# Chunked attention ahead of two MoE layers: step-by-step order on TensorE, masks made on TensorE, k and v on a second queue

## The reference

```python
def _attn_ref(q, k, v):                     # 4 batches, 8 heads, 768 tokens, 64 dims
    gamma = 1.0 - 2.0 ** (-5.0 - np.arange(H)); scale = 1.0 / np.sqrt(D)
    for t in range(S):
        state = gamma * state + outer(k[:, :, t], v[:, :, t])
        y[:, :, t] = scale * (q[:, :, t] @ state)
def _moe_ref(x, w_a, w_b, w_out):           # 3072 x 512, d_ff 1536
    return ((x @ w_a) * (x @ w_b)) @ w_out
def _moe2_ref(x, ...):                      # 8 experts, top-1 routing, d_ff 1024
    out[mask] = gate * eom * (relu(x[mask] @ w1[e]) @ w2[e])
```

## Time and profile before

| | us |
|---|---|
| median of 3 runs | 1030.78 (1030.44 to 1032.24) |
| the profiled execution | 1030.35 |
| its span, first to last instruction | 1028.5 |
| PE busy in it | 1012.5 (98%) |
| DVE, ACT, POOL busy | 553.4, 283.7, 120.2 |

### The profile page before, as it was taken

The page is one execution under the profiler, slowest core; times in us unless marked ns, Lnnn a source line. Parts: engine busy times, 40 slices in busy tenths (PEclk is TensorE's granted clock), DMA queues, the critical chain, the costliest instruction groups (busy, mean ns, idle before and its releaser), DMA issues.

```text
span 1028.5 us, 17407 instructions
## 1 busy us (share of the span) xinstructions
PE 1012.5 (98%) x5761; PEld 841.5 (82%) x5762; DVE 553.4 (54%) x1211; ACT 283.7 (28%) x490; POOL 120.2 (12%) x108
## 2 busy tenths in 40 slices
PE   6999999999999999999999999999999999999998
PEld 5898888888888888888888878888888888888886
DVE  3455342487567747773877323466554635354642
ACT  2554331221212122112211212131533424333431
POOL 4870000000000000000000000001211111211211
PEclk9999999999999999999999999999999999999999
DMA  9998700511061114103310312021754334254311
GB/s 365 368 322 264 198 1 1 144 58 46 1 158 47 41 32 133 52 31 82 93 52 21 83 41 81 2 62 41 288 178 142 134 109 164 88 175 156 114 42 37
DMA packets 53865, 114.37 MB, mean 111 GB/s; under 512 B 8749, under 2 KB 23405, under 8 KB 53296
## 3 DMA queue, kind: packets, MB, share of 16 engines
q1 hardware_dynamic: 48752, 98.95, 30.4%
q0 software_dynamic: 4480, 13.91, 4.0%
q10 hardware_dynamic: 576, 0.79, 0.2%
HBM read 96.81 MB, written 17.61 MB: 111 GB/s over the span
## 4 chain that ended last, share of the span: by engine, by line
PE 98%; DMA 1%; issue 0%; SPq 0%; DVE 0%; POOL 0%; ACT 0%; DVEq 0%; POOLq 0%
PE bank L1078 38%; PE bank L1109 19%; PE bank L1442 15%; PE bank L1466 14%; PE bank L1450 2%; PE bank L606 2%; PE bank L559 2%; PE bank L671 1%; DMA rows<-in_steps 1%; PE bank L593 1%; PE bank L573 1%; PE bank L1165 0%; PE bank L985 0%; PE bank L852 0%; PE bank L1151 0%
## 5 line engine op out<-in xcount | busy, mean ns | idle before, releaser
L1078 PE MATMUL bank<-x_hi,wab_hi 128*128 128x512 f32 x576 | 224.5, 390 | 0.0
L1078 PE MATMUL bank<-x_hi,wab_lo 128*128 128x512 f32 x576 | 224.1, 389 | 0.0
L1078 PE MATMUL bank<-x_lo,wab_hi 128*128 128x512 f32 x576 | 224.1, 389 | 0.0
L1007 DVE SCALAR_TENSOR_TENSOR products<-y_sb,gate_row 128x512 f32<-128x512 f32 x256 | 176.9, 691 | 23.7 <-DMA gate_row<-xT_dram 16.4
L1442 PE MATMUL bank<-w,xe 128*128 (+1 forms) x648 | 158.9, 399 | 0.5 <-DVE xe L695 0.5
L1442 PEld LDWEIGHTS bank<-w,xe 128*128 128x128 f32 x648 | 119.4, 188 | 28.1 <-issue 1.8
L1019 DVE TENSOR_TENSOR g_sb<-bank,b_sb 128x512 f32<-128x512 f32 x72 | 49.7, 690 | 168.2 <-PE bank L1078 168.2
L1078 PEld LDWEIGHTS bank<-x_hi,wab_hi 128*128 128x128 f32 x576 | 108.2, 188 | 22.8 <-issue 0.3
L1078 PEld LDWEIGHTS bank<-x_lo,wab_hi 128*128 128x128 f32 x576 | 108.2, 188 | 22.4
L1078 PEld LDWEIGHTS bank<-x_hi,wab_lo 128*128 128x128 f32 x576 | 108.1, 188 | 22.4
L1109 PE MATMUL bank<-wo_hi,g_hi 128*128 128x512 f32 x288 | 113.4, 394 | 0.0
(11 more groups left out here) (172 smaller groups left out, 1067.7 us busy)
## 6 DMA issues: line engine op xcount, KB each, us to landing
raw<-in_w SPq DMA_DIRECT2D x64, 512.0 KB, 6.1
gate_row<-xT_dram SPq DMA_DIRECT2D x64, 256.0 KB, 3.2
rows<-in_steps SPq DMA_DIRECT2D x20, 768.0 KB, 7.9
rows<-in_steps SPq DMA_DIRECT2D x24, 256.0 KB, 7.2
wab_raw<-in_weights SPq DMA_DIRECT2D x24, 256.0 KB, 8.5
x_rows<-y_sb SPq DMA_DIRECT2D x6, 1024.0 KB, 9.0
xT_dram<-x_all SPq DMA_DIRECT2D x4, 1024.0 KB, 11.9
x_raw<-xT_dram SPq DMA_DIRECT2D x16, 256.0 KB, 8.2
```

Source lines behind the costliest of these rows:

```text
L1007: nc.vector.scalar_tensor_tensor(products, y_sb[:, t], 1.0, gate_row[e % GATE_SLOTS], ALU.mult, ALU.mult, accum_out=L3[:, t, e:e + 1]).the ...
L1078: ins = nc.tensor.matmul(to, wab(w, f, j), x[s][:, k, :], start=(k == 0 and m == 0), stop=(k == KD - 1 and m == 2))
```

## The change

- TensorE's order in a round of steps f and s is now: scores f, kv f, scores s, within f, kv s, within s, then cross of the round. There is no look-ahead and no `first_up`; all 24 first products of the dense layer follow the last round.
- VectorE's order is now per step: probabilities, then the new state. ScalarE decays the state per step, then evicts. GpSimd's order is per step: decay k, decay q; q's buffer is taken again once the round three before is done with everything, not only with `cross`.
- kv alternates between two banks (6 and 7); the waits for slots and for v are per step.
- The masks are no longer loaded (512 KB). Two products of 4 rows by 128 and 4 rows by 512 columns make all powers of the decays in banks 4 and 5, and VectorE multiplies them with a triangle (64 KB, loaded) into `mask_t`. Before them, TensorE runs two 512-column products on zeros.
- First load: SP brings only qT and kT of the first six steps (512 KB each), ScalarE's queue k and v (512 KB each), behind the powers, the triangle and `kdec_t`; `qdec_t` goes in behind k, v of step 1. ScalarE then runs one small activation on `kdec_t`.

```diff
@@ pe_attention @@
-        scores(0, 0, True)
-        kv(0, 0, True)
         with pe.Fori(0, B) as b:
             for j in range(RB):
-                if j < RB - 1:
-                    scores(b, j + 1)
-                    kv(b, j + 1)
-                else:
-                    with pe.If(b < B - 1):
-                        scores(b, RB)
-                        kv(b, RB)
-                    with pe.If(b > B - 2):
-                        first_up()
-                cross(b, j)
-                within(b, j)
+                first, second = ROUND * j, ROUND * j + 1
+                scores(b, first)
+                kv(b, first)
+                scores(b, second)
+                within(b, first)
+                if second < CH - 1:
+                    kv(b, second)
+                within(b, second)
+                cross(b, j)
...
+        pe.wait_ge(zeros_done, 1)
+        for _ in range(2):
+            nc.tensor.matmul(bank[7], probs[0][:, 0, 0, :], probs[0][:, 0, 0:PAIRS].rearrange("p a t -> p (a t)"), start=True, stop=True)
+        for o in range(2):
+            four = slice(o * D, o * D + PAIRS)
+            pe.wait_ge(pow_in[o], 16)
+            nc.tensor.matmul(bank[4 + o], pow_t[four, 0:P], pow_t[four, P:], start=True, stop=True).then_inc(mask_made[o], 1)
@@ dve_attention @@
+        def masks():
+            dve.wait_ge(triu_in, 16)
+            for o in range(2):
+                dve.wait_ge(mask_made[o], 1)
+                nc.vector.tensor_tensor(mask_t[o], bank[4 + o].rearrange("p (a t) -> p a t", a=PAIRS),
+                                        triu.unsqueeze(1).to_broadcast([P, PAIRS, P]), ALU.mult).then_inc(mask_done, 1)
...
-                probabilities(b, j)
-                new_states(b, j)
+                for c in range(ROUND * j, ROUND * j + ROUND):
+                    probabilities(b, c)
+                    if c < CH - 1:
+                        new_state(b, c)
@@ act_attention @@
+            act.dma_start(pow_t[four], const_in[four, C_POW:C_POW + POW]).then_inc(pow_in[o], 16)
+        act.dma_start(triu, const_in[:, C_TRIU:C_QDEC]).then_inc(triu_in, 16)
+        act.dma_start(kdec_t, const_in[:, C_KDEC:C_TRIU]).then_inc(kdec_in, 16)
+        for c in range(CH):
+            kinds = slice(2 if c < CH - 1 else 3, 4)
+            act.dma_start(rows[:, c, kinds], steps_in[c][:, kinds]).then_inc(v_in[c], 16)
+            if c == 1:
+                act.dma_start(qdec_t, const_in[:, C_QDEC:C_POW]).then_inc(qdec_in, 16)
...
-                if r + 1 < ROUNDS:
-                    decayed_states((r + 1) // RB, (r + 1) % RB)
+                if ROUND * j + 1 < CH - 1:
+                    decayed_state(b, ROUND * j + 1)
+                if j < RB - 1:
+                    decayed_state(b, ROUND * j + 2)
                 evict(b, j)
@@ sp_attention @@
+        for c in range(CH):
+            sp.dma_start(rows[:, c, 0:2], steps_in[c][:, 0:2]).then_inc(qk_in[c], 16)
+        for n in range(STEPS - CH):
+            if n > 0:
+                sp.wait_ge(v_read, n)
+                load_v(n - 1 + CH)
+            if n % CH < CH - 1:
+                sp.wait_ge(kv_done, kvs_until(n))
+            else:
+                sp.wait_ge(scores_done, n + 1)
+            if n % CH > 0:
+                sp.wait_ge(q_dec_done, n // CH * (CH - 1) + n % CH)
+            load_qk(n + CH)
@@ pool_attention @@
+                if c < CH - 1:
+                    k = rows[:, c, 2].rearrange("p (h d) -> p h d", h=H)
+                    pool.wait_ge(v_in[c] if b == 0 else qk_in[c], (b + 1) * 16)
...
-                    pool.wait_ge(cross_done, r - RB + 1)
+                        pool.wait_ge(attn_done, round_no(b - 1, j) + 1 + CREDIT)
```

More of the change, by code:

```diff
@@ L407, in sp_attention @@
         load_wab(sp, 0)
-        sp.wait_ge(attn_done, ROUNDS - RB + CREDIT)
-        for i in range(ROUND):
-            load_v(ROUNDS - 1, i)
+        sp.wait_ge(v_read, STEPS - CH)
+        load_v(STEPS - 1)
         load_wo(sp, 0)
@@ new lines, in pe_attention, with scores @@
+        pe.sem_inc(state_new, CREDIT)
+        pe.sem_inc(probs_done, ROUND)
+        def scores(b, c):
+            i = c % ROUND
+            pe.wait_ge(qk_in[c], 16 * b + 16)
+            pe.wait_ge(probs_done, CH * b + c + 1)
+            qT, kT = rows[:, c, 0], rows[:, c, 1]
+            for p in range(PAIRS):
+                for o in range(2):
+                    half_p, cols = slice(o * D, (o + 1) * D), slice(p * P, (p + 1) * P)
+                    ins = nc.tensor.matmul(bank[2 * i + o][:, cols], kT[half_p, cols], qT[half_p, cols], start=True, stop=True)
+            ins.then_inc(scores_done, 1)
@@ new lines, in kv @@
+        def kv(b, c):
+            pe.wait_ge(state_new, (CH - 1) * b + max(c - 1, 0) + CREDIT)
+            pe.wait_ge(k_dec_done, (CH - 1) * b + c + 1)
+            pe.wait_ge(v_in[c], 16 * b + 16)
+            pe.sem_inc(cross_ready, 1)
+            for h in range(H):
+                p, o, cols = h // 2, h % 2, slice(h * D, (h + 1) * D)
+                ins = nc.tensor.matmul(bank[6 + c % ROUND][o * D:(o + 1) * D, p * D:(p + 1) * D],
+                                       rows[:, c, 2, cols], rows[:, c, 3, cols], start=True, stop=True)
@@ L596, in cross @@
-            ins.then_inc(cross_done, 1)
-        def within(b, j):
-            for i, c in chunks(j):
-                pe.wait_ge(probs_done, CH * b + c + 1)
-                if c == CH - 1:
-                    pe.wait_ge(v_in[c], 16 * b + 16)
-                for a in range(0, PAIRS, 2):
-                    for p, o in ((a, 0), (a + 1, 0), (a, 1), (a + 1, 1)):
-                        h = 2 * p + o
-                        ins = nc.tensor.matmul(out_at(i, p, o), rows[:, c, 3, h * D:(h + 1) * D], probs[j][:, i, h, :],
-                                               start=False, stop=(i == ROUND - 1 and p >= PAIRS - 2), skip_group_check=True)
-            ins.then_inc(attn_done, 1)
@@ L1114, in group @@
             for f in range(KF):
-                pe_up(pe, g, s, f, (0,) if first and f == 0 else (1, 0))
+                pe_up(pe, g, s, f)
                 if first and f == 0:
```

210 lines of the change are left out of this document (81 added, 129 removed).

## The result

The changed kernel takes 1037.37 us (median of 5 runs, 1036.01 to 1038.42). The kernel before, in five runs beside it, took 1030.78 us (1030.44 to 1032.24). The ratio is 1.006, with a 95% interval of 1.0045 to 1.0074: slower, by 6.6 us. The profiled execution took 1037.5 us, its span is 1035.7. Against the profile of before that is 7.2 us more.

The account below looks back on a forecast made before the run. The prediction took TensorE's order to bound the kernel, with the start waiting for DMA. Start -1.1 and steady rounds +5.2 gave +4.1 us on the profiled 1030.35, 1034.5 there and 1034.9 as median; range 1031.2 to 1039.5.

Parts of the forecast that it names:

- the steady rounds: Attention rounds 3 to 11: a batch takes 18.82 us against 17.09, three times, +5.2 us.
- The start: Up to the end of round 2: it ends at 30.3 us against 31.4, a gain of 1.1 us.
- seam: From attention to the dense layer: no gain, no loss; ScalarE may block 2 us on the first dense weights.
- the 0.21 us from the end of a VectorE instruction to TensorE: In each round: delay from the end of VectorE's probs until TensorE can use them, 0.21 us.
- forecast stall: Before a round's second within: TensorE waits 0.26 us for probs, 0.72 us in a batch's last round.
- the landing of k 0: At the start: k of step 0 lands near 9.6 us behind 384 packets, so kv 0 starts at 10.85.
- turns of one for one: In the first loads: while both DMA queues have work, they take turns packet by packet, 89 against 89.
- rival 1: At the start: second queue brings k and v in time, start gains 5.1 us, 1031.0 us, no change; chance 0.19.
- The masks by products: At the start: zeros and mask products end at 6.6 to 8.3 us, none of it on the path.
- rival 2: Steady rounds: on top of an early start, only the fifth group change is paid, 1.4 us; 1027.1 us; chance 0.07.
- rival 3: Rounds 0 and 1: TensorE may stay at 1.2 GHz, costing 2.5 to 4.5 us; 1037.4 to 1039.4 us; chance 0.13.
- Records at 62 ns from scores 0 on: At the start: sign named beforehand that TensorE's products run at 62 ns a piece from scores 0 on.

Follow-up runs that it names:

- a_extra_dve: The changed kernel with one more VectorE instruction of 128 x 512 behind the first step's work of each round 0 to 8: 1040.48 us.
- a_all_on_sp: The changed kernel with all first loads of q, k and v on SP, as in the kernel before, ScalarE's queue having only the constants: 1033.93 us.
- a_masks_loaded: The changed kernel with the two masks loaded at the head of ScalarE's queue, without powers, triangle and the products on zeros and powers: 1035.71 us.
- b_masks: The kernel before with only the masks made by products (zeros, powers, triangle); q, k and v stay on SP's queue: 1031.21 us.
- best: The changed kernel with each kind's two steps side by side, first loads on SP, `kdec_t` first, dense weights asked for sooner, low half split later: 1027.11 us.

## Why the prediction was right, and where it was off

The forecast was 1034.9 us, slower, from 1031.2 to 1039.5. The measured 1037.37 lies inside, 2.5 us above the forecast. The sum was +4.1 us on the profile, the profile shows 7.2. The direction is right by its largest term, the steady rounds. The start came out with the wrong sign, and only the width of the range holds it. By its terms:

| term | forecast | measured |
|---|---|---|
| start, to the end of round 2 | -1.1 | +1.4 |
| rounds 3 to 11 | +5.2 | +4.3 |
| seam | 0 | +0.8 |
| behind the transpose | 0 | +0.7, scatter |

**Steady rounds: mechanism right, size 0.9 too large.** Rounds of 5.88, 6.32 and 6.32 us stand against 5.98, 6.42 and 6.42. VectorE's chain sets them, as a_extra_dve shows, and scores f to probs s is as long as worked out. The term that was mis-sized is the 0.21 us from the end of a VectorE instruction to TensorE. It was read off one place at the start; here it is 49.27 - 49.21 = 0.06 us. Also, kv s between the two `within` takes 0.54 us and not 0.46, so part of the forecast stall is work.

**Start: the failed step is the landing of k 0.** The prediction counted 384 packets of ScalarE's queue up to k 0 and took the time that 384 had taken in the kernel before, 9.6 us. With the two loads of powers, 16 packets, the count is 400, which changes little. What was wrong is the pace. By 5 us ScalarE's queue had sent 16 packets, against 102 before, while SP's had sent 193 against 114; by 9 us ScalarE's had 320 against 442. The turns of one for one began only after 5 us. So `kdec_t` was there at 9.7 us, no sooner than before, with 272 packets up to it in place of 384, and k 0, 128 packets of 4 KB behind it, landed at 12.3.

The empty stretch is not a price of the half rows: a_all_on_sp, with whole rows on SP, has the same 16 packets by 5 us. With masks in place of the small loads (a_masks_loaded) ScalarE's queue had sent 143 by 5 us, and k 0, with 112 packets more ahead of it, came as late: GpSimd began at 12.44 us, against 12.40. Why the small loads leave their queue so empty stays open. With the loads on SP kv 0 comes at 10.72 us, forecast 10.85, and round 2 ends at 30.30, forecast 30.3.

That match hides two errors that cancel. In a_all_on_sp round 0 ends at 17.67 us, not 16.3, since TensorE still ran at 1.2 GHz: scores 1 took 2.08 us there, and the granted clock reads 0.50 from 10 to 14 us. (In the changed kernel's profile it reads 1.00 throughout, though scores 1 took 2.08 us there too.) And round 1 takes 6.32 us and not 7.6, since its data were there. In the changed kernel the same: kv 0 is 2.7 us late, round 0 from there 1.2 longer, round 1 1.3 shorter.

**The turns between queues** went as the rows had said: 132 packets of SP's queue to 113 of ScalarE's from 5 to 7 us, 195 to 191 from 7 to 9, 173 to 174 from 9 to 12. Only up to 5 us, with 193 to 16, ScalarE's queue lay behind. So rival 1 stayed out. The Trainium skill ("DMA: Bandwidth & Descriptors", Queues, rings and completion order) states turns of some 9 to 17 descriptors. Microsecond by microsecond the counts stay close (58 to 54, 60 to 61 and 54 to 57 from 10 to 13 us), so this trace shows nothing of such turns.

**The masks by products** were put at no cost, since kv 0 comes later anyway. Kv 0 bears that out: 13.54 us, and 13.58 with the masks loaded. The transpose was 0.7 us later with them alone on the kernel before and 1.2 later within the change, but the traces put these differences on stretches at a lower clock and on the seam (b_masks, a_masks_loaded).

**The seam: the failed step is that ScalarE "may block on them for 2 us".** It blocked 3.61 us. SP did ask for the weights as late within its order as the prediction said: at 68.31 us against 63.74 before, 4.6 later, where attention itself ran 4.3 us behind. They landed 5.0 later. Some blocking was free, as forecast, but only up to about 2.9 us; beyond that the state decay came too late, and behind it, on VectorE, the probs that TensorE needs in the same round. In `best`, where the weights are asked for sooner, only 0.24 us of idle time is left at the seam.

**Rivals.** Rival 1 (k and v in time) and rival 2 (faster) fell with the landing of k 0. Of rival 3 (clock) part came true, by another way than it said: steps of round 0 ran at 1.2 GHz (scores 1 in 2.08 us), from round 1 on none did (1.16 us), and round 0 from kv 0 on took 1.2 us longer than worked out, not 2.5 to 4.5. Its time of 1037.4 is the measured one, for other reasons.

**What was named beforehand.** Records at 62 ns from scores 0 on did not come true: scores 0 took 2.08 us, and the first dense product started at 89.31 us, not 86.8. Of the proofs of error, kv 0 came at 13.54, not before 9. The batch is within 18 to 19.5. That TensorE would wait for DMA after round 2 did come true at the seam, at second hand.

## What to carry to other kernels

Without look-ahead, put the same kinds of product of both steps side by side, so that the second step's products cover the first step's VectorE work: the batch is then as short as with look-ahead (17.07 against 17.09 us), and the start needs less data. Moving k and v to a second queue, behind constants and apart from their q, cost 3 us at the start here with the same bytes: read a row whole, or its halves back to back (kv 0 at 10.72 and 10.28 us against 13.54). When work ahead of a seam grows, look at what an in-order engine waits for there, and at all that is queued behind the wait, on the next engine too.

## What the runs showed of the hardware that I had not expected

- Order of reads: six 512 KB halves and then their other halves ran at 169 GB/s from 3 to 5 us, the same twelve in turn at 310, whole reads at 367. With masks at the head of the other queue, six halves first reached 357 in that stretch. After 7 us the changed kernel moved 407 GB/s with halves as well.
- A constant of 6 KB can come as late behind small loads as behind large ones: `kdec_t` lets GpSimd start at 9.66 us behind the 84 KB of b_masks and at 9.71 behind 512 KB, and at 5.66 us when it is first.
- Two loads of four rows at the head of ScalarE's queue: that queue had sent 16 packets by 5 us, with two loads of 128 rows 102.
- A pause can cost more than its length: in b_masks TensorE stood still for 1.34 us, the granted clock then read 0.57 for 4 us, and two rows took 1.6 us longer.
- TensorE's clock at the start differs between executions of like code. Scores 0 took 2.08 us in the changed kernel and 1.16 in a_extra_dve, whose instructions up to there are the same. It cost nothing there, since kv 0 waits for k.
- From the end of a VectorE instruction to the waiting product 0.06 us can be enough, where one place at the start had shown 0.21.
